# One block for five stages: an attention, Fourier and MLP kernel without barriers between its stages

## The reference

```python
def _attn_ref(r, k, v, w, a, b):            # state: B x H x D x D
    for t in range(S):
        y[:, :, t] = np.einsum('bhd,bhde->bhe', rt, state)
        Sa = np.einsum('bhde,bhe->bhd', state, at)
        state_decay = state * wt[:, :, None, :] - np.einsum('bhd,bhe->bhde', Sa, bt)
        state = state_decay + np.einsum('bhd,bhe->bhde', vt, kt)

def _moe_ref(x, w_ch1, w_ch2):              # x: B x S x E, hidden 1280
    mixed = np.real(np.fft.fft(np.fft.fft(x, axis=1), axis=2))
    u = x + mixed
    un = (u - mean) / np.sqrt(var + 1e-06)
    return u + np.maximum(un @ w_ch1, 0.0) @ w_ch2

def _moe2_ref(x, w_tok1, w_tok2, w_ch1, w_ch2):   # 256 and 1536 hidden
    h = np.maximum(x.transpose(0, 2, 1) @ w_tok1, 0.0) @ w_tok2
    u = x + h.transpose(0, 2, 1)
    return u + np.maximum(u @ w_ch1, 0.0) @ w_ch2
```

## Time and profile before

| | us |
|---|---|
| median of 3 runs | 1003.57 (1002.41 to 1004.55) |
| profiled execution, its time | 1002.71 |
| profiled execution, its span | 1000.9 |
| PE busy | 957.8 |
| DVE busy | 498.9 |
| ACT busy | 349.4 |
| POOL busy | 301.6 |

### The profile page before, as it was taken

The page is one execution under the profiler, slowest core; times in us unless marked ns, Lnnn a source line. Parts: engine busy times, 40 slices in busy tenths (PEclk is TensorE's granted clock), DMA queues, the critical chain, the costliest instruction groups (busy, mean ns, idle before and its releaser), DMA issues. The chain is left out here.

```text
span 1000.9 us, 48593 instructions
## 1 busy us (share of the span) xinstructions
PE 957.8 (96%) x21468; PEld 910.1 (91%) x21468; DVE 498.9 (50%) x941; ACT 349.4 (35%) x758; POOL 301.6 (30%) x361
## 2 busy tenths in 40 slices
PE   6899999999999679998999999999999999999998
PEld 3789888888988668898999999999999999999998
DVE  4366776676766347766443333444842233223322
ACT  3466565656666423322211112232321122112211
POOL 6456556656656416805200000025600000000000
PEclk9999999999999989999999999999999999999999
DMA  7366666666675336302000000003100000000000
GB/s 252 102 187 200 198 204 193 201 222 213 213 221 165 108 99 191 100 1 69 25 1 0 0 0 0 0 0 101 44 1 21 21 0 20 20 20 7 13 20 20
DMA packets 50519, 86.81 MB, mean 87 GB/s; under 512 B 6336, under 2 KB 30016, under 8 KB 50464
## 3 DMA queue, kind: packets, MB, share of 16 engines
q1 hardware_dynamic: 48848, 81.96, 26.3%
q0 software_dynamic: 880, 3.69, 1.2%
q10 hardware_dynamic: 736, 0.48, 0.2%
HBM read 70.37 MB, written 7.86 MB: 78 GB/s over the span
## 5 line engine op out<-in xcount | busy, mean ns | idle before, releaser
L1415 ACT ACTIVATE d_h_hi<-d_bank 128x384 fp32r<-128x384 f32 x96 | 47.3, 492 | 200.0 <-PE d_bank L1497 200.0
L1452 DVE SCALAR_TENSOR_TENSOR d_h_lo<-d_bank,d_h_hi 128x384 fp32r<-128x384 f32 x96 | 53.5, 558 | 78.1 <-ACT d_h_hi L1415 78.1
L1511 PE MATMUL d_bank<-w_lo,d_h_hi 128*128 128x320 f32 x288 | 89.0, 309 | 0.0
L1511 PE MATMUL d_bank<-w_hi,d_h_lo 128*128 128x320 f32 x288 | 89.0, 309 | 0.0
L1511 PE MATMUL d_bank<-w_hi,d_h_hi 128*128 128x320 f32 x288 | 89.0, 309 | 0.0
L1415 ACT ACTIVATE c_h_hi<-c_bank 128x384 fp32r<-128x384 f32 x80 | 37.5, 490 | 144.6 <-PE c_bank L1497 144.5
L1511 PE MATMUL c_bank<-w_hi,c_h_hi 128*128 128x320 f32 x240 | 74.8, 312 | 0.0
L1511 PE MATMUL c_bank<-w_hi,c_h_lo 128*128 128x320 f32 x240 | 74.2, 309 | 0.0
L1511 PE MATMUL c_bank<-w_lo,c_h_hi 128*128 128x320 f32 x240 | 74.1, 309 | 0.0
L1464 DVE TENSOR_TENSOR d_o<-d_bank,u_all 128x320 f32<-128x320 f32 x24 | 11.8, 491 | 111.1 <-PE d_bank L1511 111.1
L1452 DVE SCALAR_TENSOR_TENSOR c_h_lo<-c_bank,c_h_hi 128x384 fp32r<-128x384 f32 x80 | 42.2, 553 | 39.3 <-ACT c_h_hi L1415 39.3
(11 more groups left out here) (265 smaller groups left out, 2790.6 us busy)
## 6 DMA issues: line engine op xcount, KB each, us to landing
e_raw<-in_e SPq DMA_DIRECT2D x72, 256.0 KB, 4.3
r_raw<-in_c SPq DMA_DIRECT2D x24, 768.0 KB, 4.3
tok<-tok_of SPq DMA_DIRECT2D x24, 320.0 KB, 2.7
e_raw<-in_e SPq DMA_DIRECT2D x24, 260.5 KB, 4.1
va<-in_c SPq DMA_DIRECT2D x24, 160.0 KB, 2.5
vb<-in_c SPq DMA_DIRECT2D x24, 160.0 KB, 2.7
attention_out<-yout SPq DMA_DIRECT2D x92, 40.0 KB, 1.9
stage<-in_moe_w_ch POOLq DMA_DIRECT2D x4, 640.0 KB, 5.2
```

Of the source, the lines that this page charges most:

```text
L1415: nc.scalar.activation(h_hi[:, m, :], bank[m % 4][:, 0:TW], ACT.Relu).then_inc(h_hi_done, 1)
L1452: nc.vector.scalar_tensor_tensor(h_lo[:, m, :], bank[m % 4][:, 0:TW], 0.0, h_hi[:, m, :].bitcast(F32), ALU.max, ALU.subtract).then_inc(h_l ...
L1511: last = nc.tensor.matmul(bank[4 + t % 2][:, 0:E], lhs, rhs, start=(m == 0 and i == 0), stop=(m == NM - 1 and i == 2))
```

## The change

All stages now share one block. It is opened in `program` and handed to each stage; the engine functions of a stage are appended to it, so that an engine goes from one stage to the next by a branch, without a barrier. What the barriers covered is now waited for by name:

- `attention` returns its count of y; in the Fourier stage ACT (before the tables) and PE (before the first product) wait for the 24th y, POOL for the tables' rests and the stores.
- Each stage returns an object `Ahead`: its count of adds, the value of it at the stage's end, and its prefetch. `added` waits for the adds: PE does so before hidden tile m = 1 of every block, POOL (behind the first hidden tile) before it splits weights. `weights_split` waits until the stage before has split all its weights: SP before it fetches, PE before its loop.
- The MLP's PSUM banks change places: `bank` now takes 0 to 5 and `pre_bank` 6 and 7, where `pre_bank` had 0 and 1.
- The 14 products of `keep_busy(14)` are gone.
- The first three units of batch 0 are done by `first_pieces`, tile by tile: tiles 0 and 1 of all three units, then the last tile of all three.

```diff
@@ attention
-    blk = ctx.enter_context(nc.Block())
...
-        keep_busy(14)
+
+    return done["y"]
@@ new
+class Ahead:
...
+    def added(self, eng):
+        eng.wait_ge(self.sem, self.count)
+
+    def weights_split(self, eng):
+        eng.wait_ge(self.prefetch.lo_done, self.prefetch.parts_before(len(self.prefetch.jobs)))
@@ fourier
-        block = ctx.enter_context(nc.Block())
...
         @block.gpsimd
         def _(gp):
+            gp.wait_ge(early.tok_lo_done, 3)
+            gp.wait_ge(given.stored[0], STORED)
             gp.wait_ge(given.stored[1], STORED - 32)
...
             early.first_head(act, True, 1)
+            act.wait_ge(y_done, NG)
...
-            first(0, (0,))
+            def first_pieces():
+                pe.wait_ge(y_done, NG)
+                pe.wait_ge(early.tok_lo_done, HT)
+                pe.wait_ge(lo_done, N1)
+                pe.wait_ge(added, NA)
+                for tiles in (range(HT - 1), range(HT - 1, HT)):
+                    for n in range(3):
+                        _, f, cnt, c = first_stage(n)
+                        f0, m = KF[f]
+                        for i in tiles:
+                            x_hi, x_lo = fold_hi[:, 0, i, f0:f0 + m], fold_lo[:, 0, i, f0:f0 + m]
+                            if n == 0 and i == tiles[0]:
+                                pe.wait_ge(fold_hi_done, 3 if i else 1)
+                            for k, (lhs, rhs) in enumerate(((x_hi, tok_hi[:, i, c]), (x_hi, tok_lo[:, i, c]), (x_lo, tok_hi[:, i, c]))):
+                                if n == 0 and i == tiles[0] and k == 2:
+                                    pe.wait_ge(fold_lo_done, 3 if i else 1)
+                                last = nc.tensor.matmul(bank[n][0:m, 0:2 * cnt], lhs, rhs, start=(i == 0 and k == 0), stop=(i == HT - 1 and k == 2))
+                        if HT - 1 in tiles:
+                            last.then_inc(filled_first, 1)
+
+            first_pieces()
             for b in range(B):
-                first(b, range(1, N1))
+                first(b, range(1 if b else 3, N1))
...
+        return Ahead(added, NA * B + NA, prefetch)
@@ mlp
+        bank = [ctx.enter_context(nc.psum_tensor(f"{name}_bank{i}", [P, 512], F32)) for i in range(6)]
         pre_bank = [ctx.enter_context(nc.psum_tensor(f"{name}_pre{i}", [P, 512], F32)) for i in range(2)]
-        bank = [ctx.enter_context(nc.psum_tensor(f"{name}_bank{i}", [P, 512], F32)) for i in range(6)]
...
-        block = ctx.enter_context(nc.Block())
...
             if prefetch:
+                ahead.weights_split(sp)
                 prefetch.fetch_all(sp)
...
             def _(gp):
+                gp.wait_ge(h_filled, 1)
+                ahead.added(gp)
                 prefetch.split_all(gp, False)
...
                     elif m == 0:
                         pe.wait_ge(h_lo_done, NM * k + NM)
+                    elif m == 1:
+                        ahead.added(pe)
...
+            ahead.weights_split(pe)
             loop(pe, pre, main)
+
+        return Ahead(y_done, TB * NBLK + TB, prefetch)
```

More of the change, by code:

```diff
@@ L51, with attention @@
          "du2", "res1", "res2", "res3", "u", "ut", "ru", "rv", "rhs_v", "va", "vb", "r", "cp")
-def attention(nc, ctx, ins, consts, x_dram, following, early):
+def attention(nc, ctx, blk, ins, consts, x_dram, following, early):
     def sb(name, shape, dt=F32):
@@ L999, in fold_rest, with fourier @@
                                      ALU.subtract).then_inc(self.fold_lo_done, 1)
-def fourier(nc, given, early, norm, start, u, w_jobs):
+def fourier(nc, block, y_done, given, early, norm, start, u, w_jobs):
     with ExitStack() as ctx:
@@ L1327, in scale, with mlp @@
         last.then_inc(self.z_ready, 1)
-def mlp(nc, name, ident, u, w, hidden, norm, start, out_dram, stage, next_jobs, last_work):
+def mlp(nc, block, ahead, name, ident, u, w, hidden, norm, start, out_dram, stage, next_jobs, last_work):
     with ExitStack() as ctx:
@@ L1533, in rests, with token_mix @@
                                          ALU.subtract).then_inc(self.xl_done, 1)
-def token_mix(nc, u, w, rows, start, stage, next_jobs):
+def token_mix(nc, block, ahead, u, w, rows, start, stage, next_jobs):
     with ExitStack() as ctx:
@@ L1620, in main @@
                     c = slice(m * P, m * P + P)
+                    if m == 1:
+                        ahead.added(pe)
                     for t in range(NI):
@@ L1646, in _ @@
                 start.turn(pe, f, bank[START_BANKS[f]])
+        return Ahead(y_done, NI * B + NI, prefetch)
 class MlpWeights:
@@ L1678, in program @@
         norm = Norm(nc, sb, sem, given.second, start_c.z_ready)
+        blk = ctx.enter_context(nc.Block())
         with ExitStack() as f:
@@ L1689, in program @@
                              lambda name: c.enter_context(nc.semaphore(name)), u)
-            mlp(nc, "c", given.ident, u, w, moe_w1.shape[1], norm, start_c, None, given.stage,
+            last_c = mlp(nc, blk, last_f, "c", given.ident, u, w, moe_w1.shape[1], norm, start_c, None, given.stage,
                 token_jobs(tw, tok_w1, tok_w2) + mlp_jobs(w, ch_w1, ch_w2, tiles_c, tiles_d), rows)
-            token_mix(nc, u, tw, rows, start_d, given.stage, mlp_jobs(w, ch_w1, ch_w2, 0, tiles_c))
-        mlp(nc, "d", given.ident, u, w, ch_w1.shape[1], None, start_d, out, None, None, None)
+            last_t = token_mix(nc, blk, last_c, u, tw, rows, start_d, given.stage, mlp_jobs(w, ch_w1, ch_w2, 0, tiles_c))
+        mlp(nc, blk, last_t, "d", given.ident, u, w, ch_w1.shape[1], None, start_d, out, None, None, None)
 def constants():
```

6 lines of the change are left out of this document (4 added, 2 removed).

## The result

| | before | after |
|---|---|---|
| median, us | 1004.06 (1002.41 to 1005.78) | 995.18 (993.96 to 995.89) |
| profiled execution, its time / its span | 1002.71 / 1000.9 | 994.72 / 992.6 |
| PE busy | 957.8 | 953.8 |
| DVE / ACT / POOL busy | 498.9 / 349.4 / 301.6 | 499.6 / 349.1 / 300.6 |
| mean granted clock | 0.993 | 0.989 |

Four runs of each, on the same chip: the ratio is 0.991, with a 95% interval of 0.989 to 0.9931. The changed kernel is 8.9 us faster; 994.0 was forecast.

What follows compares the result with a forecast made beforehand. PE bounds the kernel throughout and loses time at four seams between stages: 3.3 + 2.1 + 1.25 + 1.1 = 7.75, with the clock 9.55 us. That gives 993.2 for a like execution, 994.0 us beside the median; range 991.8 to 999.2.

Steps and rivals of the forecast that it cites:

- Seam one: Attention to Fourier stage: without barrier and 14 products, and with the new tile order, unit 3 starts 3.3 us earlier.
- the clock's other side: Fourier stage's start: removing the 14 products might bring half clock there; taken as no cost, other bound 1.8 us.
- Seam two: Fourier stage to MLP c: PE starts while DVE still works, block m = 1 starts 2.1 us earlier.
- Seam three: MLP c to token stage: only the barrier is late, so PE goes on as within a stage, 1.25 us.
- Seam four: Token stage to MLP d: PE starts before DVE's last start rest has ended, 1.1 us earlier.
- The rule on increments: At the stage changes: DVE's bare increments fire once earlier work is handed out, not ended; about 0.4 us for themselves.
- The clock: First 56 products of MLP d: the fall to half clock goes, 1.8 us; bounds 0 and 1.8.
- The reasoning by gap lengths: Before MLP d: 3.3 us without ordinary products lost full clock, 2.6 before MLP c kept it; about 2.2 would keep it.
- Rival 1: The clock keeps falling behind a seam, at four or at one: only 7.75 us gained, 995.8 us; chance 0.27.
- Rival 2: At the seams, increments fire only when DVE's work has ended, with the clock still falling: 999.6 us; chance 0.10.
- rival 4: New waits in the loop bodies cost PE a gap each, 0.6 us 20 times: slower, 1006.0 us; chance 0.03.
- rival 3: Something else, as the last x tile's landing, ends last at the seams; about half the gain, 998.8 us; chance 0.08.

Runs made afterwards that it cites:

- the last experiment: The changed kernel with the already satisfied wait of m = 1 also at m = 2 and m = 3 of every MLP block: 994.92 us, ratio 0.9899.
- the changed kernel's second profile: The changed kernel measured once more without an edit, in another session: 995.26 us, ratio 0.9894 to the kernel before.

## Why the prediction was right

**Seam one, 3.3 forecast, 3.32 in the profile.** Each step held: PE waits for y, which ends 0.96 us behind the last attention product as in the earlier trace rows, and for nothing behind it, and the last tile was there in time. Two things were missing. The landing of the last tile is not "two microseconds early" in every execution (the last experiment). And the reason for which I took the clock's other side, without the 14 products, at nothing was wrong. I looked at the idle 1.0 us, but the clock had fallen already inside the last attention group, and what counts is when it comes back. With the 14 products it was back before the first Fourier product in three profiles of three. Without them it is back in time in some executions only; where it isn't, seam one gains 1.2 instead of 3.3 (8.03 against 9.22).

**What held the first barrier.** The prediction listed the 14 products among what is removed, without a price for their time. The runs give it: none, since they ended inside POOL's 1.65 us. POOL's store held the barrier, which I had not looked at, as its rows in the prediction were of other seams.

**Seam two, 2.1 against 1.89.** The increments came, as said, with DVE still at work. Only the size is off: from the flips' end to PE's start it is 0.68 us, where I had taken 0.47. On the other hand the new wait, for which I had put half a microsecond, cost nothing, since the adds ended (453.03) with the eighth product.

**Seam three, 1.25 against 1.25.** Nothing is waited for.

**Seam four, 1.1 against 1.25.** PE's start is 0.31 us behind ACT's last head (720.93), where I had taken 0.4.

**The rule on increments.** The row of MLP c's first product, 451.82, ahead of the adds' start at 452.14, shows of DVE what the earlier trace rows showed of ACT. The Trainium skill, "PSUM — Partial Sum Buffer", section "Engine vs sequencer instructions", says that such an increment can fire as soon as the instructions ahead of it are dispatched. The trace agrees, and moving the increments behind DVE's work cost 5.9 us. It is safe in this kernel because each count only opens a first round, and the data have counts of their own.

**The clock, 1.8 against 1.57.** The eight profiles of kernels that have neither the barrier nor the late increments at seam four all read 9.96 to 9.99 us for the 56 products; of the five with either of them and no filler, four read 11.53 or 11.54 and one 9.97. The reasoning by gap lengths was too fine: 2.55 us kept the clock in the kernel before, 2.55 and 2.75 did not in two others. The other side came too: half clock in the first Fourier units, in six of eleven profiles without the 14 products, two of them with PE busy across the seam. The Trainium skill, "TensorE: Matmul & The Clock Gate", section "What's actually happening", has it that activity releases the throttle; the traces agree in so far as the three profiles with the 14 products have the full clock there.

**The total.** 9.55 forecast, 9.28 in the seams' rows, 8.9 in the medians. Range and sign held. That the sum comes out so near is in part luck: the rows are of an execution whose clock was back before the first Fourier unit, and by the changed kernel's second profile they would give 7.1. Of the signs named, POOL did split from PE's second block on: its first row of the token stage starts at 679.82, where that stage starts at 676.95. Two signs of being wrong, half clock in the first units and the wait for the last tile, came in later profiles. Rival 1 was partly right: one fall went, another comes at times. Rival 2 is refuted, rival 4 as well; rival 3 appears in one execution.

## What to carry to other kernels

Price a barrier by what is late at it: follow every engine to its last step ahead of it, DMA issues included, and not only the engine that is busy last. Then ask for each count what its increment really stands behind: an increment without work attached runs ahead of the work before it, which is time gained where the count only opens a round, and a race where it stands for data. Where PE bounds a kernel, look behind each gap at what the next products take, since here, behind a gap of some 2 us, the next 56 products took 1.6 us longer in four profiles of five. And before filler products are taken out as idle work, look at the granted clock behind them: they can cost nothing and still be of use.

## What the runs showed of the hardware

- A barrier opened 1.65 us behind a DMA issue that ended last on POOL (371.20 to 372.85), 0.65 behind one that ended last on SP (378.81 to 379.46), and 0.3 behind the end of DVE's last operation.
- Behind one barrier, 14 products that compute nothing left the clock whole for the next stage's first products (27 products in 4.83 us in the kernel before), and without them these ran at half clock (6.74 us from 373.14).
- DVE's sequencer ran at least two 320-column adds ahead of the engine (451.82 against 452.14).
- Half clock is not bound to one place: behind gaps of nearly equal length it came or stayed away, and the kernel before varied from 1000 to 1012 us over the sessions, the changed one from 994 to 998. A difference of under 2 us between two kernels needs more than one profile.
